# The first layers of the second MLP as seven block products instead of eight

## The reference

```python
def _moe_ref(x, w1, w2, w3, w_out):
    a = x @ w1
    b = x @ w2
    h = a * b @ w3
    return h @ w_out

def _moe2_ref(x, w1, w2, w3, w_out):
    h = np.maximum(np.maximum(x @ w1, x @ w2), x @ w3)
    return h @ w_out
```

## Time and profile before

| | us |
|---|---|
| median of 3 runs (725.23 to 726.4) | 725.72 |
| the profiled execution, its time | 725.54 |
| the profiled execution, its span in the trace | 723.8 |
| PE busy | 713.2 |
| DVE busy | 219.8 |
| ACT busy | 193.0 |
| POOL busy | 210.9 |

### The profile page before, as it was taken

One profiled execution on the slowest core, in us unless ns is written; L12 is line 12 of the kernel. 1 busy time (PEld: TensorE's weight loads), 2 busy tenths in 40 slices (PEclk: granted clock), 3 DMA queues, 4 the chain that ended last, 5 costly groups with the idle time before them and its releaser, 6 DMA issues.

```text
span 723.8 us, 14645 instructions
## 1 busy us (share of the span) xinstructions
PE 713.2 (99%) x6560; PEld 595.1 (82%) x6560; DVE 219.8 (30%) x392; ACT 193.0 (27%) x417; POOL 210.9 (29%) x186
## 2 busy tenths in 40 slices
PE   6999999999999999999999999999999999999998
PEld 4778788888888888888888998888888888888898
DVE  3464554414453345411100455111111111111111
ACT  5465423322332233312221533111120112111110
POOL 5799423303232223321220231130122114011210
PEclk9999999999999999999999999999999999999999
DMA  9874122202221121122000320000001000000100
GB/s 321 264 233 142 53 74 74 74 24 75 74 75 54 54 92 58 40 80 81 1 1 0 117 73 1 1 35 24 1 0 60 1 0 25 34 1 1 43 16 29
DMA packets 18590, 43.57 MB, mean 60 GB/s; under 512 B 2144, under 2 KB 2912, under 8 KB 18528
## 3 DMA queue, kind: packets, MB, share of 16 engines
q1 hardware_dynamic: 18528, 42.64, 18.2%
HBM read 37.91 MB, written 4.72 MB: 59 GB/s over the span
## 4 chain that ended last, share of the span: by engine, by line
PE 97%; DMA 1%; POOL 1%; SPq 1%; ACT 0%; DVE 0%; issue 0%
PE psum L346 30%; PE psum L348 29%; PE psum L347 29%; PE psum L385 2%; PE psum L363 2%; PE psum L356 2%; PE psum L394 1%; PE psum L373 1%; DMA attention<-ident 1%; POOL weights_split L738 1%; SPq L310 0%; POOL acts_split L738 0%; ACT attention L622 0%; DVE psum L528 0%; DVE psum L533 0%
## 5 line engine op out<-in xcount | busy, mean ns | idle before, releaser
L346 PE MATMUL psum<-acts_split,weights_split 128*128 128x512 f32 (+1 forms) x992 | 370.3, 373 | 0.6 <-POOL weights_split L738 0.6
L348 PE MATMUL psum<-acts_split,weights_split 128*128 128x512 f32 (+1 forms) x992 | 366.0, 369 | 0.0
L347 PE MATMUL psum<-acts_split,weights_split 128*128 128x512 f32 (+1 forms) x992 | 365.8, 369 | 0.0
L346 PEld LDWEIGHTS psum<-acts_split,weights_split 128*128 128x128 f32 x992 | 187.0, 188 | 34.6 <-issue 2.6
L348 PEld LDWEIGHTS psum<-acts_split,weights_split 128*128 128x128 f32 x992 | 187.0, 189 | 31.7
L347 PEld LDWEIGHTS psum<-acts_split,weights_split 128*128 128x128 f32 x992 | 187.1, 189 | 30.1
L738 POOL TENSOR_TENSOR acts_split<-gate,acts_split 128x512 fp32r<-128x512 f32 (+1 forms) x70 | 82.5, 1179 | 438.0 <-ACT acts_split L622 438.0
L622 ACT ACTIVATE acts_split<-gate 128x512 fp32r<-128x512 f32 (+1 forms) x70 | 41.2, 589 | 246.9 <-DVE gate L608 152.0
L622 ACT ACTIVATE gate<-psum 128x512 f32<-128x512 f32 (+1 forms) x70 | 38.8, 555 | 130.3 <-PE psum L348 130.3
L738 POOL TENSOR_TENSOR acts_split<-xy,acts_split 128x512 fp32r<-128x512 f32 (+1 forms) x44 | 52.2, 1207 | 55.7 <-ACT acts_split L622 55.7
L582 DVE TENSOR_TENSOR gate<-gate,psum 128x512 f32<-128x512 f32 (+1 forms) x40 | 25.4, 634 | 129.0 <-PE psum L348 129.0
(11 more groups left out here) (42 smaller groups left out, 378.4 us busy)
## 6 DMA issues: line engine op xcount, KB each, us to landing
xy<-wa SPq DMA_DIRECT2D x40, 256.0 KB, 5.4
attention<-qk SPq DMA_DIRECT2D x16, 576.0 KB, 4.2
attention<-v_win SPq DMA_DIRECT2D x16, 384.0 KB, 3.4
attention<-wb SPq DMA_DIRECT2D x24, 256.0 KB, 3.0
attention<-v_down SPq DMA_DIRECT2D x16, 320.0 KB, 3.2
out_t<-attention SPq DMA_DIRECT2D x16, 256.0 KB, 2.0
out_t<-attention SPq DMA_DIRECT2D x4, 128.0 KB, 1.7
attention<-mask SPq DMA_DIRECT2D x1, 96.0 KB, 5.7
```

What stands on the lines that cost most here:

```text
L346: pe.matmul(out, lhs[:, 0], rhs[:, 0], start=first, stop=False)
L347: pe.matmul(out, lhs[:, 0], rhs[:, 1], start=False, stop=False)
L348: return pe.matmul(out, lhs[:, 1], rhs[:, 0], start=False, stop=last)
```

## The change

The first layers of the second MLP are computed by Strassen's method in its form with 7 products and 15 additions. A superblock is 768 tokens (three of them), seen as two halves of 384 tokens; two tiles f of one weight matrix and two tiles k of channels make a 2 x 2 block of weights, and two k tiles and two token halves a 2 x 2 block of activations. A unit is such a pair of f for one of w1, w2, w3 (9 units in a superblock), and has seven products, each over two pairs of k (`KP`), of three matmuls of 384 columns. The products are accumulated over k in three PSUM banks a unit, some on top of others (P2 on P1; P7 and P4 on P6; P3 on P5); `p16`, `c22`, `c21`, `c12`, `c11` on DVE form the sums, `raise_top` the maxima over w1, w2, w3. `split_h2` on ACT and POOL splits the results. The fourth layer is plain, eight output tiles of 384 columns a superblock, six f each, three matmuls.

The seven combined weights of each block are made in block 3 of the first MLP, from position 205 on, every 2 positions, in 18 steps n: SP loads a raw piece of 256 KB (`load_raw`), ACT copies it to PSUM (COPY_RAW), DVE makes the sums (COMBINE, four operations of 128 columns), ACT the high parts (HIGH_WB, 896 columns), DVE the low parts (LOW_WB), and SP stores both, 896 KB, to DRAM (`store_ready`). Six more steps do the same for w_out without sums, storing 512 KB. There are two buffers for each of these. Later each unit's weights (1.8 MB) are loaded into a ring of four (`load_unit`), again in every superblock. The activations' differences (`make_y`, DVE) and their splits (`split_y`, ACT and POOL) are made for superblock 0 during the second layer of the last block, and for the others beside the fourth layer before them.

The core of the diff:

```diff
+def preparations(late):
+
+    return [PROLOGUE + PARTS * 2 + 45 + 2 * n + late for n in range(PREPS)]
...
+            load_raw(0)
+            load_raw(1)
+            for n in range(PREPS):
+                store_ready(n)
+                if n + 2 < PREPS:
+                    load_raw(n + 2)
             for i in range(2):
-                sp.wait_ge(out_stored[i], 16 * NB * JO // 2)
+                sp.wait_ge(made_out[i], 16 * PREPS // 2)
+            for u in range(RING):
+                sp.wait_ge(mlp_done, GROUPS * (NB - 1) + (8, 14, 16, 16)[u])
+                load_unit(u)
+            sp.wait_ge(mlp_done, GROUPS * NB)
+            sp.dma_start(wo_t[:, :].bitcast(F32), wo_dram).then_inc(wo_in, 16)
...
+            def pair_product(u, e):
+                s, before = u // UPS, u - 2
+                a, b, c = pair_banks(u)
+                out = {1: a, 2: a, 6: b, 7: b, 4: b, 5: c, 3: c}[e]
...
+                elif e == 2:
+                    pe.wait_ge(p1_taken, u + 1)
+                elif e == 7:
+                    pe.wait_ge(p16_ready, u + 1)
+                elif e == 4:
+                    pe.wait_ge(p167_ready, u + 1)
+                elif e == 3:
+                    pe.wait_ge(c22_ready, u + 1)
...
+                for kp in range(KP):
+                    if u % UPS == 0:
+                        pe.wait_ge(y_lo, 7 * KP * s + Y_SPLIT[(e, kp)] + 1)
+                    mm = split_product(out, ring[u % RING][:, kp, :, LHS[e], :], y_r[(e, kp)],
+                                       kp == 0 and e in (1, 5, 6), kp == KP - 1, True)
+                mm.then_inc(l3_done, 1)
...
+            def combine(n):
+                if n >= UPS * KP:
+                    return
+                made = made_b[n % 2].rearrange("p (e c) -> p e c", e=8)
+                raw = raw_b[n % 2].rearrange("p (e c) -> p e c", e=4)
+                dve.wait_ge(raw_copied, n + 1)
+                dve.tensor_tensor(made[:, 1, :], made[:, 7, :], raw[:, 2, :], ALU.add).then_inc(s1_made, 1)
+                dve.tensor_tensor(made[:, 3, :], made[:, 4, :], raw[:, 3, :], ALU.subtract)
+                dve.wait_ge(s1_made, n + 1)
+                dve.tensor_tensor(made[:, 2, :], made[:, 1, :], raw[:, 0, :], ALU.subtract).then_inc(s2_made, 1)
+                dve.wait_ge(s2_made, n + 1)
+                dve.tensor_tensor(made[:, 0, :], raw[:, 1, :], made[:, 2, :], ALU.subtract).then_inc(s_made, 1)
...
+                                 [(at, ("COMBINE", n)) for n, at in enumerate(preparations(0.5))],
+                                 [(at, ("LOW_WB", n)) for n, at in enumerate(preparations(1.3))],
...
+            def copy_raw(n):
+                if n < 2:
+                    act.wait_ge(x_ready, UNITS)
+                ge(act, wb_lo, n - 1)
+                act.wait_ge(wb_in[n % 2], 16 * (n // 2 + 1))
+                copy(made_b[n % 2][:, DM:], raw_b[n % 2]).then_inc(raw_copied, 1)
...
+                                 [(at, ("COPY_RAW", n)) for n, at in enumerate(preparations(0))],
+                                 [(at, ("HIGH_WB", n)) for n, at in enumerate(preparations(1))],
```

More of the change, by code:

```diff
@@ L148, in after_parts, with first_activations, pair_products, done @@
     return [x for x in out if x[1][0] in kinds]
-def second_weights(late):
-    at = PROLOGUE + PARTS * (NB - 1) + late
-    return [(at + 17 + 16 * (f // 2) + 1.8 * (4 * (f % 2) + m), ("SPLIT_WB", f, m)) for f in range(4) for m in range(4)]
+def preparations(late):
+    return [PROLOGUE + PARTS * 2 + 45 + 2 * n + late for n in range(PREPS)]
+def first_activations(late):
+    at = PROLOGUE + PARTS * (NB - 1) + 4 * F1 + 0.6 + late
+    return [(at + 0.55 * i, step) for i, step in enumerate(Y_STEPS)]
+def pair_products():
+    out = []
+    for u in range(UPS):
+        out += [(u, 1), (u, 6)]
+        if u:
+            out += [(u - 1, 4), (u - 1, 3)]
+        out += [(u, 5), (u, 2), (u, 7)]
+    return out + [(UPS - 1, 4), (UPS - 1, 3)]
+DONE = {ue: i + 1 for i, ue in enumerate(pair_products())}
+def done(u, e):
+    return 7 * UPS * (u // UPS) + DONE[(u % UPS, e)]
+def later(u):
+    return 2 * (u // 3) + u % 3
 def in_order(*lists):
@@ L343, in _, with split_product @@
+            for i in range(2):
+                sp.wait_ge(out_stored[i], 16 * SUPER * JO)
         @block.tensor
         def _(pe):
[L345 to L348, removed]
+            def split_product(out, lhs, rhs, first, last, read_between=False):
+                pe.matmul(out, lhs[:, 0], rhs[:, 0], start=first, stop=False, skip_group_check=read_between)
+                pe.matmul(out, lhs[:, 0], rhs[:, 1], start=False, stop=False, skip_group_check=read_between)
+                return pe.matmul(out, lhs[:, 1], rhs[:, 0], start=False, stop=last, skip_group_check=read_between)
@@ L596, in _, with p16 @@
                 run[step[0]](*step[1:])
[L598 to L617, removed]
+            def p16(u):
+                _, b, _ = pair_banks(u)
+                dve.wait_ge(p1_taken, u + 1)
+                dve.wait_ge(l3_done, done(u, 6))
+                dve.tensor_tensor(p16_sb[u % 2], p1_sb[u % 2], b, ALU.add).then_inc(p16_ready, 1)
@@ new lines, in raise_top, with c11 @@
+            def raise_top(u, top, value, value_ready, count):
+                dve.wait_ge(value_ready, u + 1)
+                ge(dve, count, later(u) - 1)
+                dve.tensor_tensor(top, top, value, ALU.max).then_inc(count, 1)
+            def c11(u):
+                a, _, _ = pair_banks(u)
+                top = tops[u // 3 % 2][0]
+                dve.wait_ge(c11_copied, u // 3 + 1)
+                dve.wait_ge(l3_done, done(u, 2))
+                ge(dve, top11, later(u) - 1)
+                dve.tensor_tensor(top, top, a, ALU.max).then_inc(top11, 1)
@@ new lines, in c22 @@
+            def c22(u):
+                _, b, c = pair_banks(u)
+                top = tops[u // 3 % 2][3]
+                to = p167_sb if u % 3 else top
+                dve.wait_ge(l3_done, done(u, 7))
+                if u == 0:
+                    dve.wait_ge(y_lo, 7 * KP)
+                if u % 3 == 0:
+                    ge(dve, h2_lo, 4 * (u // 3 - 1))
+                if u % UPS == 1:
+                    ge(dve, out_stored[1], 16 * JO * (u // UPS))
+                dve.tensor_tensor(to, p1_sb[u % 2], b, ALU.add).then_inc(p167_ready, 1)
+                dve.wait_ge(p167_ready, u + 1)
+                dve.tensor_tensor(to, to, c, ALU.add).then_inc(c22_ready, 1)
+                if u % 3:
+                    raise_top(u, top, to, c22_ready, top22)
@@ new lines, in high_wb, with split_y @@
+            def high_wb(n):
+                full, width = (made_b[n % 2], PART_W) if n < UPS * KP else (made_b[n % 2][:, DM:], DM)
+                if n < UPS * KP:
+                    act.wait_ge(s_made, n + 1)
+                else:
+                    act.wait_ge(raw_copied, n + 1)
+                ge(act, made_out[n % 2], 16 * (n // 2))
+                copy(ready_b[n % 2][:, 0:width].bitcast(F32R), full[:, 0:width]).then_inc(wb_hi, 1)
+            def split_y(s, e, kp):
+                if Y_SPLIT[(e, kp)] == 0 and s == 0:
+                    act.wait_ge(y_ready, 2 * JO)
+                    act.wait_ge(mlp_done, GROUPS * (NB - 1) + 2 * F1)
+                    for i in range(2):
+                        act.wait_ge(made_out[i], 16 * PREPS // 2)
+                if e >= 4:
+                    act.wait_ge(y_made, 4 * KP * s + Y_MADE[({5: 1, 6: 2, 7: 3, 4: 4}[e], kp)] + 1)
+                if s:
+                    act.wait_ge(l3_done, done(UPS * s - 1, e))
+                copy(y_r[(e, kp)][:, 0, :], y_source(s, e, kp)).then_inc(y_hi, 1)
@@ new lines, in copy_out @@
+            def copy_out(s, g):
+                act.wait_ge(l4_done, 2 * JO * s + g + 1)
+                ge(act, out_stored[g % 2], 16 * (JO * s + g // 2))
+                copy(out_sb[g % 2], bank(l4_bank(s, g))[:, 0:HALF]).then_inc(out_ready, 1)
+            for s in range(SUPER):
+                for u in range(UPS * s, UPS * (s + 1)):
+                    take_p1(u)
+                    if u % UPS and u % 3 == 0:
+                        split_h2(u - 1)
+                    if u % 3 == 0:
+                        copy_c11(u)
+                split_h2(UPS * (s + 1) - 1)
+                steps = [(1.7 * i, ("E", e, kp)) for i, (kind, e, kp) in enumerate(Y_STEPS)
+                         if kind == "E" and s + 1 < SUPER]
+                outs = [(15.5 + (1.05 * g if g < 5 else 4.2 + 3.1 * (g - 4)), ("OUT", g)) for g in range(2 * JO)]
+                for step in in_order(steps, outs):
+                    if step[0] == "E":
+                        split_y(s + 1, *step[1:])
+                    else:
+                        copy_out(s, step[1])
@@ L820, in layouts @@
     uo = np.asarray(i["moe2_w_out"]).reshape(F2, P, JO, P)
[L821 removed]
+    wb = []
+    for fp in range(FP):
+        for u in (u1, u2, u3):
+            for k in range(0, KD, 2):
```

(3 more changed lines are left out.)

372 lines of the change are left out of this document (239 added, 133 removed).

## The result

The changed kernel takes 740.49 us (739.92 to 741.78, 4 runs) against 725.71: ratio 1.0205, 95% interval 1.0188 to 1.0223. It does fewer matmul columns and is slower by 1.9 to 2.2%. Its profiled execution took 741.78 us, the slowest of the four, with a span of 740.0, 16.2 more than the 723.8 of before.

The account below looks back on a forecast made before the run. The prediction took PE's matmuls, number times pitch, to bound the kernel. It summed 723.8 - 24.3 + 37.1 + 0.2 = 736.8 us span, plus 1.74 around it, to 738.5 us, range 729 to 744 (chance 0.54).

Parts of the forecast that it names:

- PE's saving: Second MLP's matmuls on PE: third layer 221.8 to 196.5 us, fourth 73.9 to 74.9, a gain of 24.3 us.
- the seam: Start of the second MLP: superblock 0's activation splits ready during the second layer before it, costing 0, at most 2 us.
- rival D: Second MLP's 384-column matmuls: pitch 0.189 us, the weight load, instead of 0.1733; 25 us more, 763 us; chance 0.03.
- The strict order: MLP 1's block 3: ACT and DVE run as written, so late preparations delay GATE and H, and PE waits.
- The cycle: Block 3's preparations: a pair takes 10.2 us, 5.0 from LOW to landing and 5.2 on engines, against 5.44 planned.
- The engines' part: Block 3: from a raw piece's landing to LOW of an odd preparation, COPY through LOW on ACT and DVE, 5.2 us.
- The walk: Block 3's preparations followed from first loads at 319.77 us to COMBINE 17's end at 408.05 and last h at 410.8.
- The stall: Block 3's last h: ready at 410.8 us where PE used it at 373.7 before, so PE stands 37.1 us.
- My sign for it: PE idle between 330 and 411 us, released by block 3's ACT or DVE work and POOL's last low, 37 us.
- Rival A: SP's queue in block 3: load not held by the store, landing 3.05 us, stall 21.5, total 722.9; chance 0.20.
- Rival B: Block 3: the chain is much shorter than added up or slack swallows it, total 701.4 us; chance 0.09.
- Rival C: Second MLP: the combination chain on DVE also makes PE wait, 13.5 us over 27 units, total 752; chance 0.14.

Follow-up runs that it names:

- The fastest version: The changed kernel with four raw buffers, wider pace, LOW_WB behind the next COMBINE, two activation splits moved later, and stores in halves: 703.06 us, ratio 0.9691.
- the seam's move: Against a kernel with four raw buffers, wider pace and LOW_WB reordered: ACT splits products 4 and 3's activations after the first MLP's last output copies; 707.87 us.

## Why the prediction was right, point by point

- **PE's saving.** Forecast 24.3 us. The pitch came out as interpolated, and the second MLP took 273.4 us including the 1.63 us of the seam, 271.8 without, against my 271.4. The fastest version ends 723.8 - 701.5 = 22.3 us earlier than the kernel before, with the seam's 1.1 us and the later start of the stretch (320.1 against 319.8) in it. The bound of 0.189 (rival D) is out; the weight loads beside 384-column matmuls are hidden like the others.
- **The strict order turns the chain into PE's wait.** Shown by PE's waits of 15.0 and 12.1 us, and by their going as the chain is shortened or moved. The two that I named (gate product, low part of h) are the ones.
- **The cycle.** Forecast 10.2 us, measured 9.73 to 9.81 for six pairs and 11.27 for one, whose load took 5.7 us; the mean is 9.97. Its largest term, 5.0 us from LOW to landing, held: LOW ends 390.44, COPY starts 395.33, 4.89 us. The engines' part was 0.35 too long, most of it COMBINE (0.93 and not 1.2). The walk's last gate product was at 408.05 and came at 406.66. One reading was loose: with eleven loads in flight the queue moved 216 to 417 GB/s and not 250 to 417; no term rests on it.
- **The stall.** Forecast 37.1, measured 34.7. My sign for it, PE idle for 37 us, did not come: PE is idle for 27.1, since its matmuls in between run at the lower clock.
- **What I had left out** made up for it, and that is luck: the clock, 2.6 us in the rest of block 3, where PE ran at 1.2 GHz for 5.3 us after its longest wait; and 1.05 us before the stretch (the first `wb` issue comes at 319.8 before, at 319.6 to 322.4 in the versions above, and at 320.1 and 320.6 in two executions of the version with halved stores: it varies from execution to execution). With the seam's 1.6 and 0.4 in the second MLP these are 5.7 us against the 2.4 of the stall; so the profiled execution is 3.2 us above my 738.5 and the median 2.0. A forecast that lets PE stand must add what its clock costs.
- **Seam.** Forecast 0, at most 2: 1.63. The step missed is that ACT's output copies stand behind splits that wait for DVE and POOL: the copy at 467.00 comes behind two splits that waited 2.07 and 0.76 us for the last two differences on DVE, which took 2.64 us with POOL busy.
- **Rival A** (the load passes the store) was false in the change, and the experiment that put the load first landed at 725.65, where I had worked out 722.9 for a landing of 3.05. **Rival B** (nothing stalls) was false for this kernel and is what the better schedule reaches: 703.06 against 701.4. **Rival C** didn't come: the view of PE's waits from 468 to 737 us is empty.

So the products are worth 3.1% (703.06), and their first schedule more than took it away. Of the 37.4 us between 740.49 and 703.06, four raw buffers alone give 21.3 (the order of two issues alone 14.8) and the wider pace alone 20.5 (719.99). They overlap, for both shorten or move the same chain: together they give 35.1 (705.42). Halved stores and the seam's move give the last 1.6 to 2.4. (The kernel before took 725.32 to 725.97 us on the chips of these runs, so single steps of half a microsecond say nothing.)

## What to carry to other kernels

When work is moved beside a loop whose engines run in a written order, compare its chain per piece, DMA landings included, with the pace at which it is planned; the sum of busy times (DVE was 44% busy) says nothing. A prefetch with two buffers that is issued behind a large store on the same queue landed after that store here: issue it first or one stage earlier. And where a buffer is held by its store, start the store as early as its first half is ready.

## What the runs showed of the hardware

- A 256 KB load right behind an 896 KB store on one queue landed 4.4 us after its issue, ahead of it 3.0, with no store beside it 2.6. The store landed after 4.1 us ahead of the load and 4.7 behind it.
- After 8.78 us of waiting PE's 512-column matmuls had a pitch of 0.43 us for 5.3 us, then 0.2267 again. Waits of 3.52, 4.17 and 4.08 us were followed by the same pitch for 2.7, 5.3 and 2.7 us; after those of 1.51, 1.68 and 3.34 us it was 0.23 from the second matmul on.
- 384-column fp32r matmuls, each with a weight load of its own, had a pitch of 0.1736 us.
- DVE operations of 384 columns with two SBUF sources took 0.92 us each beside a busy POOL (two in 1.84 us, from 456.71) or 1.32 (two in 2.64, from 463.48), and 0.56 with POOL idle (at 486.63). With one source in PSUM it was 0.55 though POOL was at work (at 487.60). The Trainium skill (SBUF — State Buffer, SBUF: two separate sides) has the two engines take turns at a shared port for a whole instruction when the DVE one has two SBUF inputs; the numbers agree.
